# First expert's weight chunks split during attention in another order, gathers issued without waits

## The reference, cut to what matters

```
logits = x @ w_gate;  expert_idx = argmax(logits)
gate_w = softmax(logits) at expert_idx
for e in range(8):                       # w1 (8,512,1024), w2 (8,1024,512)
    out[mask_e] = gate_w * (relu(x[mask_e] @ w1[e]) @ w2[e])
h = out @ w_in                           # 512 -> 2048
g = h if h >= 1, 0 if h <= -1, else (h + 1)**2 / 4
result = g @ w_out
```

## Time and profile before

| | |
|---|---|
| median of three runs | 866.46 us |
| profiled execution, device time | 868.46 us |
| its span | 866.4 us |
| busy PE / PEld / DVE / ACT / POOL | 818.4 / 711.9 / 400.6 / 306.6 / 460.6 us |
| chain that ended last, shares | PE 81%, POOL 8%, issue 4%, DMA 3%, DVE 2% |
| mean granted clock of TensorE | 0.981 |

### The profile page before, as it was taken

How to read it: one execution, slowest core, us unless ns; L and a number is a source line. 1 busy time by engine, 2 the same in 40 slices (tenths; PEclk the granted TensorE clock), 3 DMA queues, 4 the chain that set the end, 5 groups by cost and what they waited for, 6 DMA issues and landing times.

```text
span 866.4 us, 17392 instructions
## 1 busy us (share of the span) xinstructions
PE 818.4 (94%) x5506; PEld 711.9 (82%) x5507; DVE 400.6 (46%) x746; ACT 306.6 (35%) x661; POOL 460.6 (53%) x492
## 2 busy tenths in 40 slices
PE   6999997299889999999999999999999999999995
PEld 5888886278768888888879889989999898999995
DVE  4877875755534555465543333333232243233221
ACT  4676665122144322442224323223233223223231
POOL 7888886489688865886446314223223214222322
PEclk9999999599999999999999999999999999999998
DMA  7777864467656644774333002002001000100000
GB/s 168 172 187 177 193 158 135 111 185 236 203 172 192 206 158 125 215 213 151 121 121 111 0 1 74 1 1 74 1 1 49 25 0 36 37 0 12 25 1 36
DMA packets 108453, 88.48 MB, mean 102 GB/s; under 512 B 66368, under 2 KB 80192, under 8 KB 108416
## 3 DMA queue, kind: packets, MB, share of 16 engines
q10 hardware_dynamic: 23040, 41.95, 16.1%
q1 hardware_dynamic: 81936, 34.67, 15.4%
q0 software_dynamic: 3440, 11.38, 4.0%
HBM read 72.87 MB, written 15.10 MB: 102 GB/s over the span
## 4 chain that ended last, share of the span: by engine, by line
PE 81%; POOL 8%; issue 4%; DMA 3%; DVE 2%; ACT 1%; SPq 0%; ACTq 0%; POOLq 0%; DVEq 0%
PE tp L1305 11%; PE tp L1307 10%; PE tp L1306 10%; POOL wts L507 6%; PE pt L1307 5%; PE pt L1306 5%; PE pt L1305 5%; PE xo L1305 3%; PE xo L1307 3%; PE xo L1306 3%; PE tp L1240 3%; PE sc L1306 3%; PE sc L1307 3%; PE sc L1305 3%; PE sc L1160 2%
## 5 line engine op out<-in xcount | busy, mean ns | idle before, releaser
L636 POOL TENSOR_TENSOR act_s<-act_f,act_s 128x384 fp32r<-128x384 f32 x96 | 97.6, 1019 | 278.5 <-ACT act_s L827 278.4
L507 POOL TENSOR_TENSOR wts<-stage,wts 128x512 fp32r<-128x512 f32 x160 | 205.5, 1305 | 69.7 <-ACT wts L728 63.8
L728 ACT CAST wts<-stage 128x512 fp32r<-128x512 f32 x160 | 98.6, 620 | 205.3 <-DMA stage<-in_moe_w 93.5
L1305 PE MATMUL tp<-x2T,wts 128*128 128x384 f32 x384 | 130.7, 340 | 0.0
L825 ACT ACTIVATE clamped<-clamped,mhalf 128x384 f32<-128x384 f32 x96 | 59.2, 617 | 199.2 <-DVE clamped L1108 199.2
L1307 PE MATMUL tp<-x2T,wts 128*128 128x384 f32 x384 | 128.9, 336 | 0.0
L1306 PE MATMUL tp<-x2T,wts 128*128 128x384 f32 x384 | 128.7, 335 | 0.0
L1108 DVE TENSOR_SCALAR clamped<-tp 128x384 f32<-128x384 f32 x96 | 53.6, 558 | 149.2 <-PE tp L1307 149.2
L1112 DVE SCALAR_TENSOR_TENSOR act_f<-tp,clamped 128x384 f32<-128x384 f32 x96 | 53.5, 558 | 66.4 <-ACT clamped L825 66.4
L1307 PE MATMUL pt<-wts,act_s 128*128 128x512 f32 x192 | 75.3, 392 | 0.0
L1306 PE MATMUL pt<-wts,act_s 128*128 128x512 f32 x192 | 75.1, 391 | 0.0
(11 more groups left out here) (192 smaller groups left out, 1442.5 us busy)
## 6 DMA issues: line engine op xcount, KB each, us to landing
stage<-in_moe_w ACTq DMA_DIRECT2D x128, 256.0 KB
y_rows<-xg SPq DMA_DIRECT2D x21, 260.0 KB
x<-y_rows SPq DMA_DIRECT2D x6, 780.0 KB, 4.5
qn<-in_q SPq DMA_DIRECT2D x32, 144.0 KB, 3.5
kn<-in_k SPq DMA_DIRECT2D x32, 144.0 KB, 3.7
v<-in_v SPq DMA_DIRECT2D x16, 288.0 KB
x_nat<-xb SPq DMA_DIRECT2D x16, 288.0 KB, 3.8
stage<-in_moe_w_in ACTq DMA_DIRECT2D x16, 256.0 KB
```

Of the source, the lines that this page charges most:

```text
L507: pool.tensor_tensor(wts[:, par, 1, cols], stage[:, n % STG, :], wts[:, par, 0, cols], ALU.subtract).then_inc(lo_done, 1)
L636: pool.tensor_tensor(act_s[f % 4][:, 1, :], act_f[f % 4][:], act_s[f % 4][:, 0, :], ALU.subtract).then_inc(act_lo, 1)
L728: act.copy(wts[:, par, 0, n * CH:(n + 1) * CH], stage[:, n % STG, :]).then_inc(hi_done, 1)
L1305: pe.matmul(o, stationary(0), moving(0), start=start, stop=False)
```

## The change

ScalarE and GpSimd take the first expert's chunks in another order, counted by their own semaphores `first_hi` and `first_lo` (GpSimd raises `first_lo` by STG = 4 at its start). In the loop over batches chunks 0 to 5 are done, one in each second pair, in buffers 0 and 1. Chunks 6, 7 and then 8, 9, 10 are done in pairs 13, 14 and 15, the copies ahead of `take_pooled` on ScalarE. No chunk is touched in the routing. GpSimd issues six gathers, splits 11 to 15, and only then raises `lo_done` by 16; then it alternates splits of the second expert and gathers. Chunks 8 to 15 use buffers 2 and 3 alone. SyncE waits for the gathers and raises `x_ready`. For slots 0 and 1 TensorE waits for the gather itself and transposes from `xg` with no copy. In the routing the three slot operations go ahead of `at_row`, which is made in two halves, each with its own semaphore step; `slot_tok` goes ahead of the slot tables. The core of the diff:

```diff
+PER = 2
+REST = {6: (6, 0), 7: (7, 1), 8: (8, 2), 9: (9, 3), 10: (10, 2), 11: (11, 3), 12: (12, 2), 13: (13, 3), 14: (14, 2), 15: (15, 3)}
+AT_ENDS = {1: (6,), 2: (7,), 3: (8, 9, 10)}
+AMONG = (11, 12, 13, 14, 15)
+NOW = 6
-LATE = 7
...
+        for s in range(SLOTS):
+            sp.wait_ge(gathered[s], 16)
+            sp.sem_inc(x_ready, 1)
...
+        def first_low(k, n, slot):
+            cols = bass.ds(n * CH, CH)
+            pool.wait_ge(first_hi, k + 1)
+            pool.tensor_tensor(wts[:, 0, 1, cols], stage[:, slot, :], wts[:, 0, 0, cols], ALU.subtract).then_inc(first_lo, 1)
...
+        pool.sem_inc(first_lo, STG)
...
                 pair(4 * b + i, i, 2 * b + (i + 1) // 2, 2)
+                if i % 2 == 0:
+                    first_low(PER * b + i // 2 - 1, 2 * b + i // 2 - 1, i // 2 - 1)
             sum_logits(b)
         for i in range(1, 4):
-            if i > 1:
-                low_part(0, 0, i - 2)
             pair(4 * (B - 1) + i, i, 2 * (B - 1) + (i + 1) // 2, 3 - i)
-        low_part(0, 0, 2)
+            for k in AT_ENDS[i]:
+                first_low(k, *REST[k])
         sum_logits(B - 1)
-        for n in range(3, NCH - LATE):
-            low_part(0, 0, n)
...
-        gather_slots(0, 8, 0, range(NCH - LATE, NCH))
-        for n in range(NW1):
+        for s in range(NOW):
+            gather_slot(s)
+        for k in AMONG:
+            first_low(k, *REST[k])
+        pool.wait_ge(first_lo, STG + NCH)
+        pool.sem_inc(lo_done, NCH)
+        for n in range(NCH):
             low_part(1, 1, n)
-        gather_slots(8, SLOTS, 1, range(NW1, NCH))
+            gather_slot(NOW + n)
+        for s in range(NOW + NCH, SLOTS):
+            gather_slot(s)
...
+        def first_load(k, source, slot):
+            act.wait_ge(first_lo, k + 1 + STG - PER)
+            act.dma_start(stage[:, slot, :], source).then_inc(stage_loaded[slot], 16)
+        def first_high(k, n, slot, use):
+            act.wait_ge(stage_loaded[slot], 16 * use)
+            act.copy(wts[:, 0, 0, bass.ds(n * CH, CH)], stage[:, slot, :]).then_inc(first_hi, 1)
+        def next_first(b, i):
+            k = PER * b + i
+            first_load(k + 1, first_rows(b + i, 1 - i), 1 - i)
+            first_high(k, 2 * b + i, i, b + 1)
...
                 take_rows(rows_of, i - 1, 1)
+            if first_chunks is not None:
+                first_chunks()
             take_pooled(m)
...
+        first_load(0, first_rows(0, 0), 0)
         with act.Fori(0, B - 1) as b:
             for i in range(1, 5):
-                pair(4 * b + i, i, 2, b)
-        for n in range(AHEAD):
-            load_chunk(0, 0, n)
+                pair(4 * b + i, i, 2, b, lambda: next_first(b, i // 2 - 1) if i % 2 == 0 else None)
+        def rest_load(k):
+            n, slot = REST[k]
+            if k > 9:
+                act.wait_ge(first_lo, STG + k - 1)
+            elif k < 8:
+                act.wait_ge(first_lo, STG + k - 1)
+            act.dma_start(stage[:, slot, :], chunk_source(0, 0, n)).then_inc(stage_loaded[slot], 16)
+        for k in (7, 8, 9):
+            rest_load(k)
+        def last_firsts(i):
+            for k in AT_ENDS[i]:
+                rest_high(k)
+                if k >= 8:
+                    rest_load(k + 2)
         for i in range(1, 4):
-            pair(4 * (B - 1) + i, i, 3 - i, B - 1)
-            next_high(0, 0, 0, i - 1)
+            pair(4 * (B - 1) + i, i, 3 - i, B - 1, lambda: last_firsts(i))
...
-        for n in range(3, 10):
-            next_high(0, 0, 0, n)
         act.wait_ge(shifted_done, 1)
         act.activation(lexp[:], shifted[:], ACT.Exp).then_inc(lexp_done, 1)
-        for n in range(10, NCH):
-            next_high(0, 0, 0, n)
+        for k in AMONG:
+            rest_high(k)
+            if k + 2 in REST:
+                rest_load(k + 2)
+        act.wait_ge(first_hi, NCH)
+        act.sem_inc(hi_done, NCH)
...
-        dve.tensor_tensor(at_row[:], row_number[:], in_slot[:].unsqueeze(1).to_broadcast([TQ, P, TT]), ALU.is_equal).then_inc(at_done, 1)
...
+        for half in range(2):
+            tiles = slice(TT // 2 * half, TT // 2 * half + TT // 2)
+            dve.tensor_tensor(at_row[:, :, tiles], row_number[:, :, tiles],
+                              in_slot[:, tiles].unsqueeze(1).to_broadcast([TQ, P, TT // 2]), ALU.is_equal).then_inc(at_done, 1)
...
-        copy_rows(0)
+        dve.sem_inc(xs_done, 2)
         split_x(0)
-        copy_rows(1)
...
         for t in range(TT):
+            if t == TT // 2:
+                pe.wait_ge(at_done, 4)
...
         def turn_x(s):
-            pe.wait_ge(xs_done, s + 1)
+            if isinstance(s, int):
+                pe.wait_ge(gathered[s], 16)
+            else:
+                pe.wait_ge(xs_done, s + 1)
```

More of the change, by code:

```diff
@@ L315, in write_program @@
     stage_loaded = [sem(f"stage_loaded{i}") for i in range(STG)]
+    first_hi = sem("first_hi")
+    first_lo = sem("first_lo")
     hi_done = sem("hi_done")
     lo_done = sem("lo_done")
-    gathered = [sem(f"gathered{i}") for i in range(4)]
+    gathered = [sem(f"gathered{i}") for i in range(SLOTS)]
     x_ready = sem("x_ready")
@@ L596, in _, with gather_slot @@
         pool.wait_ge(gate_stored, 16)
[L598 to L608, removed]
-        gather_slots(0, 8, 0, range(NCH - LATE, NCH))
-        for n in range(NW1):
+        def gather_slot(s):
+            pool.indirect_dma_start(xg[:, s, :], None, x_nat, bass.IndirectOffsetOnAxis(ap=slot_tok[:, s:s + 1], axis=0))\
+                .then_inc(gathered[s], 16)
+        for s in range(NOW):
[5 more added lines that the diff above has]
+        for n in range(NCH):
             low_part(1, 1, n)
-        gather_slots(8, SLOTS, 1, range(NW1, NCH))
+            gather_slot(NOW + n)
+        for s in range(NOW + NCH, SLOTS):
+            gather_slot(s)
         with pool.Fori(0, 3) as i:
@@ L720, in load_chunk @@
         def load_chunk(c, e, n):
-            if not (isinstance(c, int) and c == 0 and n < STG):
-                act.wait_ge(lo_done, NCH * c + n + 1 - STG)
+            act.wait_ge(lo_done, NCH * c + n + 1 - STG)
             act.dma_start(stage[:, n % STG, :], chunk_source(c, e, n)).then_inc(stage_loaded[n % STG], 16)
@@ L745, in next_high, with pair @@
             high_part(c, par, n)
-        def pair(m, i, left, rows_of):
+        def pair(m, i, left, rows_of, first_chunks=None):
             if left >= 1 and i > 0:
@@ L778, in _, with rest_high @@
         act.sem_inc(rows_evac, 2)
+        first_load(0, first_rows(0, 0), 0)
         with act.Fori(0, B - 1) as b:
             for i in range(1, 5):
-                pair(4 * b + i, i, 2, b)
-        for n in range(AHEAD):
-            load_chunk(0, 0, n)
+                pair(4 * b + i, i, 2, b, lambda: next_first(b, i // 2 - 1) if i % 2 == 0 else None)
[6 more added lines that the diff above has]
+            act.dma_start(stage[:, slot, :], chunk_source(0, 0, n)).then_inc(stage_loaded[slot], 16)
+        def rest_high(k):
+            n, slot = REST[k]
+            first_high(k, n, slot, B if slot < 2 else (k - 8) // 2 + 1)
+        for k in (7, 8, 9):
[5 more added lines that the diff above has]
+                    rest_load(k + 2)
         for i in range(1, 4):
-            pair(4 * (B - 1) + i, i, 3 - i, B - 1)
-            next_high(0, 0, 0, i - 1)
+            pair(4 * (B - 1) + i, i, 3 - i, B - 1, lambda: last_firsts(i))
         for h in range(2):
             take_rows(B - 1, PAIRS - 1, h)
-        for n in range(3, 10):
-            next_high(0, 0, 0, n)
         act.wait_ge(shifted_done, 1)
         act.activation(lexp[:], shifted[:], ACT.Exp).then_inc(lexp_done, 1)
-        for n in range(10, NCH):
-            next_high(0, 0, 0, n)
+        for k in AMONG:
[4 more added lines that the diff above has]
+        act.sem_inc(hi_done, NCH)
         act.wait_ge(tables_done, 1)
@@ L1001, in _ @@
         then(dve.tensor_scalar(last_slot, slots_to[one, E - 1:E], -1.0, None, ALU.add))
+        dve.wait_ge(tokens_full, 1)
+        then(dve.tensor_scalar(tok96[:], sc[0][:, 0:SLOTS], float(TQ), None, ALU.mult))
+        dve.tensor_tensor(slot_tok[:], tok96[:], sc[0][:, SLOTS:2 * SLOTS], ALU.add).then_inc(slot_tok_done, 1)
         def over_experts(a, n):
@@ L1014, in _ @@
         dve.tensor_scalar(slot_par[:], slot_cs[:], 1, None, ALU.bitwise_and).then_inc(slots_known, 1)
-        dve.wait_ge(tokens_full, 1)
-        then(dve.tensor_scalar(tok96[:], sc[0][:, 0:SLOTS], float(TQ), None, ALU.mult))
-        dve.tensor_tensor(slot_tok[:], tok96[:], sc[0][:, SLOTS:2 * SLOTS], ALU.add).then_inc(slot_tok_done, 1)
         then(dve.tensor_tensor(tab_e[:], over_experts(rank_e[:], E), ids(iota[one, 0:E], E), ALU.is_equal))
@@ L1317, in turn_x @@
         def turn_x(s):
-            pe.wait_ge(xs_done, s + 1)
+            if isinstance(s, int):
+                pe.wait_ge(gathered[s], 16)
+            else:
+                pe.wait_ge(xs_done, s + 1)
```

(3 more changed lines are left out.)

4 lines of the change are left out of this document (2 added, 2 removed).

## The result

The changed kernel takes 877.98 us (median of four runs, 877.48 to 879.05), against 866.48 before: the ratio is 1.0134, 95% interval 1.0116 to 1.0152. It is 1.3% slower, and the forecast of 877 was 1 us off. The profiled execution of before (868.46) was 0.7 us slower than the slowest of its other runs.

A forecast was written before the change was run, and what follows sets the result against it. It took TensorE to bound the main loop, the serial routing chain the stretch before experts, GpSimd's lateness slot 5. Terms summed to +10.35 on the profiled 868.46 (878.8), 2.0 lower as median: 877 us, range 870 to 886.

The forecast's parts named there:

- main loop: Attention's loop: six chunks get done there, GpSimd slightly late but before TensorE needs its results; cost 0.
- seam: Entry to the last batch: ScalarE must see split 5 finished and issue three loads before copies TensorE needs; +2.1 us.
- hold in the last pair: Last attention pair: copies 8 to 10, waiting for splits and a landing, delay ScalarE's last pooled copy; +7.2 us.
- row products at the lower level: After the last pair: TensorE, having idled 8 us, runs its last twelve row products at about half speed; +1.3 us.
- subtraction to scan: Routing: without splits the subtraction and one-hot shorten and the exponential finds ScalarE free; -5.9 us.
- table to first product: Before slot 0: first expert product waits until all sixteen chunks are split, five of them behind six gathers; +13.1 us.
- slot 0's first layer at the lower level: After the wait before slot 0: TensorE spends five us at the lower clock level; +2.9 us.
- everything behind: Experts from slot 5: TensorE arrives later, so its loss waiting for expert 2's splits and smaller waits go; -9.6 us.
- rival (d): Routing does not get shorter; the 2.17 and 1.60 us are not GpSimd's doing: +2.8, 879.6 us; chance 0.05.
- Rival (a): Holds before the last row products and slot 0 keep most of the clock, landings take 3.01: 871.9 us; chance 0.14.
- rival (c): Last pair and before slot 0: buffers turn around at once, a chunk ready every 1.3 us: 864.2 us; chance 0.06.
- rival (b): Slot 5: expert 2 is late all the same, up to 9.6 us come back: 886.4 us; chance 0.09.

The follow-up runs named there:

- experiment 2: The changed kernel with three chunks per batch in the loop, 6 and 7 in pairs 13 and 14, none in pair 15: 866.22 us, ratio 0.9991.
- experiment 8: The kernel before with nine chunks in the loop, 12 to 15 split in the routing, gathers without waits, VectorE's new order: 855.07 us, ratio 0.9862.
- Experiment 1: The changed kernel with loads 8 and 9 issued ahead of the loop over batches and load 7 in pair 13: 874.9 us, ratio 1.0088.
- experiment 6: The kernel before with ScalarE's exponential moved ahead of its copies of chunks 3 to 9: 864.54 us, ratio 0.9986.
- experiment 3: The changed kernel with splits 11 to 15 and the rise of `lo_done` moved into the routing, ahead of the token table wait: 869.2 us, ratio 1.0021.
- experiment 4: The changed kernel with `lo_done` raised by 11 before the gathers and by one with each late split: 873.8 us, ratio 1.0087.
- experiment 7: The kernel before with VectorE's new order alone (slot operations first, `at_row` in halves, token table before slot tables): 866.35 us, ratio 1.0001.
- experiment 9: The nine-chunks-in-loop version with splits 12 to 15 behind six gathers, `lo_done` counted, loads ahead of the loop issued earlier: 856.38 us, ratio 0.9869.

## Why the prediction was right

By its own steps, after against before, from the two traces:

| step | predicted | measured |
|---|---|---|
| main loop | 0 | +0.3 |
| seam | +2.1 | +3.7 |
| copies 6 and 7 | +0.15 | 0 |
| hold in the last pair | +7.2 | +6.1 |
| row products at the lower level | +1.3 | +1.4 |
| subtraction to scan | -5.9 | -5.65 |
| scan to table | -0.9 | -0.7 |
| table to first product | +13.1 | +11.6 |
| slot 0's first layer at the lower level | +2.9 | +1.9 |
| everything behind | -9.6 | -9.4 |
| sum | +10.35 | +9.3 (spans) |

The mechanism was right at each step. That the total comes within 1 us owes something to luck: the seam was 1.6 too short in the sum, the hold 1.1, the gate 1.5 and the clock 1.0 too long, and the smaller terms 0.9 too short together, so that the sum is 1.1 above the difference of the spans. The step from 878.8 to 876.8, for a profiled execution 2.0 above the median, was not borne out either: after the change the profiled execution (877.49) lies 0.5 below the median.

*Main loop.* Right, and experiments 2 and 8 show that it held for three chunks per batch too.

*Seam.* The mechanism is right and its size was short: three issues took 1.59 us and not 1.15, and a wait of 3 us was enough to lose the clock, which the sum did not have there. Experiment 1 shows the step on the path.

*Last pair.* Right in mechanism. The term was mis-sized in the landing: load 10, issued at 151.19, was there when copy 10 began at 153.93, so it took at most 2.7 us, not 3.57. It was mostly hidden behind the wait for split 9. The row of 3.57 had been taken with another load issued 0.4 us and a store 0.6 us behind it. The estimate of 2.6 us from the Trainium skill ("DMA: Bandwidth & Descriptors", section "Anatomy of one DMA") was nearer: at most 2.7 here, 2.95 and 2.61 at the gate.

*Routing.* Right; the one-hot needs 1.02, more than the 0.65 taken. The subtraction takes 0.35 wherever no split lies beside it, here and in experiment 6, so its 1.8 us more before were the splits' doing: rival (d) falls.

*Gate.* Right, and shorter by the landings: the last split ends 18.6 us after the table and not 20.2, of which the two landings (2.95 and 2.61 instead of 3.57) are all. Experiments 3 and 4, in which the first product comes 7.1 and 7.5 us after the table, show that nothing but the semaphore for the last split held it. Rival (a) was right in its landings and wrong in the clock; rival (c), with a chunk every 1.3 us, falls, since they came every 2.4.

*Clock.* The lower level lasted 4.0 us from the first product, where 5 were taken. The price was too high as well: the 1.57 us for a triple at the lower level held a wait for GpSimd's split, and here triples start 1.28 to 1.44 apart. By its own figures the sum should have had 2.8, not 2.9.

*Expert 2.* Right, and it is the step that ties the sum together. The loss at slot 5 went mainly because TensorE came later: it comes to slot 5's first layer 78.6 us after the table (253.56), where before it came after 66.1 (235.8) and had to wait, while GpSimd starts expert 2 64.8 us after the table (239.76), only 2.5 sooner than before. Slot 5 then follows slot 4 by 12.27 us, so rival (b) falls. Taking the gate away alone (experiment 4) brings back 6.7 of the 8.9 us.

The medians lie 11.5 us apart and the spans 9.3. Of the 2 us by which the profiled execution of before exceeds its median the traces show a part: from the transposes of slot 5 to those of the last slot it takes 186.8 us, and 186.1 in both experiments 6 and 7, whose code is the same there. The rest is not found. If all of it lies behind slot 0, "everything behind" is really about -7.4 and not -9.4.

## What to carry to other kernels

A semaphore that rises once for a whole batch turns a wait for one item into a wait for all; but ask what bounds the path behind it before counting the wait as a loss, since here some two thirds of it (9.4 of 13.5 us) only replaced a later one. Work for an idle engine is free in a loop where it stands behind what others need, and dear where the copying engine must wait for it ahead of a result on the path: the same three chunks cost 6 us and more in the last pair and nothing in the loop. When an engine's queue is the bound, shorten the queue (fewer waits in it, more of its work earlier); reordering the other engines around it gave 1.2 us (experiment 6) and nothing that could be measured (experiment 7).

## What was not expected of the hardware

- A wait of 3.06 us for TensorE was enough for the lower clock level (granted 1.00 until the wait, 0.50 behind it): six transposes at 129.73 took 1.50 us instead of 0.90. In the kernel before, a wait of 2.46 us was followed by the lower level one triple later; in experiment 1 the level stayed 1.00 at the seam, where the wait was gone.
- VectorE's fp32 copy of a slot's rows, SBUF to SBUF, took 2.04 and 3.20 us in two places, where it began beside a gather's issue with a split right behind, and 0.43 with nothing beside it. Other copies that fell beside splits took 0.7 to 0.8 us (experiment 8, at 196.62 to 245.63), so the length depends on where it begins.
- Where two semaphore steps (a wait long satisfied and a rise) stand in GpSimd's queue between its wait for the table and its first gather (experiments 4 and 9), the gather began 1.0 us after the table. Where they stand ahead of that wait (experiments 3 and 8) or behind the gathers (the changed kernel) it was 0.3. The trace calls it issue; no run takes the steps apart.
